# The first unit's gates in two parts, on VectorE instead of GpSimd, with new positions for the start of a fused attention and MLP kernel

## The reference

```python
scale = np.minimum(mag, 0.999) / (mag + 1e-06)          # mag = |a_re + i a_im|
for t in range(S):                                      # S = 768 steps, 4 batches, 8 heads, D = 48
    S = a[t] * S + k[t] (x) v[t]                        # complex state, D x D per head
    y[t] = q[t] . Re(S)
...
h = x @ w_in                                            # 3072 x 384 @ 384 x 2048
g = np.where(h > 0.0, h, np.exp(np.minimum(h, 0.0)) - 1.0)
x = g @ w_out
h = np.maximum(np.maximum(x @ w1, x @ w2), x @ w3)      # 384 -> 768, three times
return h @ w_out2                                       # 768 -> 384
```

## Time and profile before

| | us |
|---|---|
| median of 3 runs (931.10 to 932.78) | 932.74 |
| the profiled execution | 932.65 |
| its span | 930.9 |
| PE busy in the span | 847.4 (91%) |
| DVE, ACT, POOL busy | 517.6, 419.5, 373.0 |

### The profile page before, as it was taken

The page is one execution under the profiler, slowest core; times in us unless marked ns, Lnnn a source line. Parts: engine busy times, 40 slices in busy tenths (PEclk is TensorE's granted clock), DMA queues, the critical chain, the costliest instruction groups (busy, mean ns, idle before and its releaser), DMA issues.

```text
span 930.9 us, 14390 instructions
## 1 busy us (share of the span) xinstructions
PE 847.4 (91%) x5692; PEld 734.5 (79%) x5692; DVE 517.6 (56%) x702; ACT 419.5 (45%) x613; POOL 373.0 (40%) x272
## 2 busy tenths in 40 slices
PE   0067789899999999999999999999999999999997
PEld 0067789888888888888878888878888989898987
DVE  4858887788797878787878643553212121212020
ACT  6745746466666666666575423432121121112121
POOL 3544654444545454636454522465222131303120
PEclk9997898899999999999999999999999999999999
DMA  5396143435252625262524326003010102000000
GB/s 223 88 281 195 35 123 105 139 104 176 84 167 60 202 64 182 63 205 61 174 78 147 107 59 247 1 1 119 1 69 0 68 1 69 1 35 1 35 0 35
DMA packets 70723, 88.45 MB, mean 95 GB/s; under 512 B 15360, under 2 KB 55296, under 8 KB 70144
## 3 DMA queue, kind: packets, MB, share of 16 engines
q1 hardware_dynamic: 70656, 87.53, 30.1%
HBM read 59.13 MB, written 28.39 MB: 94 GB/s over the span
## 4 chain that ended last, share of the span: by engine, by line
PE 74%; issue 9%; DVE 7%; POOL 5%; ACT 3%; DMA 1%; POOLq 0%; SPq 0%; DVEq 0%; ACTq 0%
PE bank L1123 73%; POOL t L514 1%; DVE ge L862 1%; DVE t L868 1%; ACT t L633 1%; DVE t L862 1%; PE bank L1138 1%; POOL gl L517 1%; DVE qp L868 1%; POOL hl L517 1%; DVE ge L865 1%; POOL wol L517 1%; POOL qd L514 1%; POOL kd L514 1%; DVE kp L868 0%
## 5 line engine op out<-in xcount | busy, mean ns | idle before, releaser
L517 POOL TENSOR_TENSOR gl<-ge,gh 128x512 fp32r<-128x512 f32 x96 | 131.1, 1366 | 146.1 <-ACT gh L633 146.1
L868 DVE TENSOR_TENSOR hm<-bank,hm 128x512 f32<-128x512 f32 x72 | 49.8, 692 | 226.6 <-PE bank L1123 224.7
L1123 PE MATMUL bank<-xh,wih 128*128 128x512 f32 (+1 forms) x336 | 126.9, 378 | 9.7 <-DVE xl L868 9.7
L517 POOL TENSOR_TENSOR hl<-hm,hh 128x512 fp32r<-128x512 f32 x36 | 46.5, 1292 | 205.8 <-ACT hh L633 205.8
L1123 PE MATMUL bank<-gh,woh 128*128 128x512 f32 (+1 forms) x336 | 124.2, 370 | 5.2 <-POOL gl L517 4.8
L1123 PE MATMUL bank<-xh,wal 128*128 128x512 f32 x324 | 126.2, 389 | 0.0
L1123 PE MATMUL bank<-xl,wah 128*128 128x512 f32 x324 | 126.2, 389 | 0.0
L1123 PE MATMUL bank<-xh,wah 128*128 128x512 f32 x324 | 126.1, 389 | 0.0
L1123 PE MATMUL bank<-xh,wil 128*128 128x512 f32 (+1 forms) x336 | 122.2, 364 | 0.0
L1123 PE MATMUL bank<-xl,wih 128*128 128x512 f32 (+1 forms) x336 | 122.0, 363 | 0.0
L1123 PE MATMUL bank<-gl,woh 128*128 128x512 f32 (+1 forms) x336 | 121.6, 362 | 0.0
(11 more groups left out here) (83 smaller groups left out, 1681.8 us busy)
## 6 DMA issues: line engine op xcount, KB each, us to landing
q_cols<-qp SPq DMA_DIRECT2D x24, 384.0 KB, 2.8
k_cols<-kp SPq DMA_DIRECT2D x24, 384.0 KB, 3.0
qt<-q_cols SPq DMA_DIRECT2D x24, 384.0 KB, 3.7
kt<-k_cols SPq DMA_DIRECT2D x24, 384.0 KB, 3.9
vv<-in_v SPq DMA_DIRECT2D x12, 448.0 KB, 5.5
ar<-in_a_re SPq DMA_DIRECT2D x12, 384.0 KB, 3.6
ai<-in_a_im SPq DMA_DIRECT2D x12, 384.0 KB, 4.2
qd<-in_q SPq DMA_DIRECT2D x12, 384.0 KB, 4.2
```

Of the source, the lines that this page charges most:

```text
L517: return nc.gpsimd.tensor_tensor(dst, whole, high.bitcast(f32), ALU.subtract)
L868: return nc.vector.tensor_tensor(dst, a, b, op)
L1123: return nc.tensor.matmul(dst, lhsT, rhs, start=start, stop=stop)
```

## The change

Unit 0's gate steps are done for row a and row b apart, on 128x384 tiles, each with its own semaphores, and the four steps that were POOL's are DVE's for them. A part p counts these: parts 0 and 1 are unit 0's rows, part u + 1 is unit u. Part 0 leaves ACT's arctan table without `back()`, part 1 enters without the explicit load; before each `exps` of unit 0 a load stands in the built program all the same. Unit 0's gates are loaded by row. Row b's rotated q and k go to `qp2` and `kp2`. Tables of positions: new ones for units 0 and 1, own ones for part 1, unit 2 and unit 3, and small changes for the rest; 8 positions fewer lie ahead of group 0.

```diff
+    AT_FIRST_B = {
...
+    BY_UNIT = (AT_FIRST, AT_SECOND, AT_THIRD, AT_FOURTH, AT)
...
+    START = 8
...
-        def gates(u):
-            return second if u == 1 else usual
+        def gates(p):
+            if p < PAIR:
+                return Gates(*(t[:, p:p + 1, :] for t in usual))
+            return second if p == PAIR else usual
...
+        def q_turned(n):
+            return qp2[:, :, :] if n == 1 else qp[:, :, :]
...
-                    return STEPS + EARLY * k // (2 * C1)
+                    return START + (STEPS + EARLY - START) * k // (2 * C1)
...
+                if u == 0:
+                    sp.dma_start(gates(p).ar, a_re[0, :, p:p + 1, :]).then_inc(l_first[p], 16)
+                    sp.dma_start(gates(p).ai, a_im[0, :, p:p + 1, :]).then_inc(l_first[p], 16)
...
-                nc.scalar.preload_act_table(ACT.Sin)
-                act.wait_ge(tan, u + 1)
+                if p != 1:
+                    nc.scalar.preload_act_table(ACT.Sin)
+                of_gate(act, tan1, tan, p)
                 func(g.t2, g.t2, ACT.Arctan).then_inc(atn, 1)
-                back()
...
+                if p != 0:
+                    back()
...
+            def decayed(n):
+                e, u = place_of(n), unit_of(n)
+                g = gates(part_of(n))
+                dve.wait_ge(dec, part_of(n) + 1)
+                dve.wait_ge(l_q[u % 2], 16 * (u // 2 + 1))
+                tt(g.qd[:, e, :], g.qd[:, e, :], g.cs[:, e, :], ALU.mult).then_inc(qkd1, 1)
...
-                if n >= 1:
+                if n >= 2:
                     dve.wait_ge(s_q, 16 * n)
```

More of the change, by code:

```diff
@@ L55, in build @@
     AT = {
[L56 to L59, removed]
+        "square": -21, "square_im": -22, "squared": -20, "root": -17, "denominator": -17, "inverse": -13, "clamp": -15,
@@ L60, in build @@
+        "log_decay": -15, "signed": -8, "tangent": -13, "arctan": -9, "angle": -8, "scan_lam": -10, "center": -9, "exps": -7,
+        "ends": -5, "scan_phi": -7, "reduced": -6, "decayed_a": -10, "decayed_b": -8, "sines": -4, "rotate_q_a": -3,
+        "rotate_k_a": -4, "rotate_q_b": 2, "rotate_k_b": 5, "state_decay": 3, "s_a": 6, "s_b": 10, "kr_a": 7, "kr_b": 11,
         "masked_a": 6, "masked_b": 10, "kr_evac_a": 6, "kr_evac_b": 11, "state_decayed_a": 6, "state_decayed_b": 8, "y_a": 8,
-        "y_b": 11, "inc_a": 10, "inc_b": 14, "state_add_a": 10, "state_add_b": 14, "x_high_a": 9, "x_low_a": 9, "x_high_b": 12,
@@ L65, in build @@
+        "load_kt_a": 7, "store_q_b": 7, "load_qt_b": 8, "store_k_b": 8, "load_kt_b": 8, "store_ends": -6, "load_ends": -4,
+        "tile": 13, "negative": -13, "small": -15,
     }
     AT_FIRST = {
-        "square": -26, "square_im": -25, "squared": -36, "root": -24, "denominator": -29, "inverse": -21, "clamp": -23,
-        "log_decay": -20, "signed": -20, "tangent": -21, "arctan": -20, "angle": -17, "scan_lam": -20, "center": -18,
-        "exps": -16, "ends": -15, "scan_phi": -16, "reduced": -16, "decayed_a": -17, "decayed_b": -15, "sines": -15,
@@ L76, in build @@
-        "store_k_b": -12, "load_kt_b": -4, "store_ends": -16, "load_ends": -12, "tile": 5, "negative": -20, "small": -21,
+        "square": -52, "square_im": -52, "squared": -48, "root": -46, "denominator": -47, "inverse": -42, "clamp": -39,
+        "log_decay": -38, "signed": -36, "tangent": -40, "arctan": -38, "angle": -36, "scan_lam": -38, "center": -36,
+        "exps": -34, "ends": -28, "scan_phi": -33, "reduced": -31, "decayed_a": -33, "decayed_b": -31, "sines": -31,
+        "rotate_q_a": -28, "rotate_k_a": -27, "rotate_q_b": -25, "rotate_k_b": -25, "state_decay": -8, "s_a": -22, "s_b": -18,
@@ L77, in build @@
+        "small": -42,
+    }
+    AT_FIRST_B = {
+        "square": -50, "square_im": -49, "squared": -47, "root": -42, "denominator": -43, "inverse": -40, "clamp": -38,
+        "log_decay": -37, "signed": -33, "tangent": -38, "arctan": -33, "angle": -32, "scan_lam": -35, "center": -35,
+        "exps": -32, "ends": -22, "scan_phi": -30, "reduced": -29, "sines": -30, "load_a": -49, "negative": -41, "small": -40,
     }
     AT_SECOND = {
-        "square": -39, "square_im": -37, "squared": -38, "root": -34, "denominator": -34, "inverse": -34, "clamp": -31,
@@ L81, in build @@
[L81 to L85, removed]
@@ new lines, in build @@
+        "log_decay": -37, "signed": -27, "tangent": -41, "arctan": -28, "angle": -27, "scan_lam": -28, "center": -26,
+        "exps": -26, "ends": -25, "scan_phi": -26, "reduced": -24, "decayed_a": -25, "decayed_b": -24, "sines": -5,
+        "rotate_q_a": -5, "rotate_k_a": -5, "rotate_q_b": -1, "rotate_k_b": -2, "state_decay": 0, "s_a": 3, "s_b": 6, "kr_a": 5,
+        "kr_b": 8, "masked_a": 4, "masked_b": 7, "kr_evac_a": 5, "kr_evac_b": 9, "state_decayed_a": -5, "state_decayed_b": 1,
+        "y_a": 6, "y_b": 10, "inc_a": 7, "inc_b": 8, "state_add_a": 7, "state_add_b": 12, "x_high_a": 7, "x_low_a": 7,
@@ L937, in reduced, with scan_phi @@
+            def scan_phi(p):
+                g = gates(p)
+                dve.wait_ge(phi, p + 1)
+                dve.wait_ge(gsum, p + 1)
+                nc.vector.tensor_tensor_scan(flat(g.t3), starts(p), flat(g.t2), 0.0, ALU.mult, ALU.add).then_inc(psum, 1)
+            def reduced(p):
+                g = gates(p)
+                dve.wait_ge(psum, p + 1)
                 ts(g.t2, g.t3, 4.0 * MAGIC, ALU.add, 4.0 * MAGIC, ALU.subtract).then_inc(turn, 1)
-                dve.wait_ge(turn, u + 1)
```

415 lines of the change are left out of this document (255 added, 160 removed).

## The result

The changed kernel takes 936.27 us (median of 4 runs, 935.90 to 937.88), the kernel before, beside it on the same chip, 931.92. The ratio is 1.0053, with a 95% interval of 1.0040 to 1.0066. Forecast was 919.5, with a range of 909 to 928. The profiled execution of the changed kernel took 937.88 us, its span 936.1: it is the longest of the four, 1.6 us above their median, so a difference between two traces is sure to a us or two, and the medians decide.

The account below looks back on a forecast made before the run. Only the start, ahead of group 16, was taken to have much to give, set by the units' chains. Group 16 at 188.0, plus 729.5 behind it and 1.75 outside the span, made 919.2, stated as 919.5 us; range 909 to 928.

Parts of the forecast that it names:

- Unit 0's chain: From unit 0's gates to its first scores: these at 38.2 us, 10.2 us earlier, with ACT the longer queue.
- Group 0 at 55.9: Start of group 0 on PE: 17.7 us behind the first scores, 22.4 us earlier than before.
- PE idle ahead of group 2 for 7 to 11 us: Sign to look for in the changed trace: PE waits this long, released by DVE's elu of group 0.
- Unit 1's scores at 84.6: Scores of unit 1 on PE: 2.3 us later than before, with its gates' second half ahead of group 0's elu.
- the 82 that I named as a sign of error: Unit 1's rotations on DVE: the prediction called itself wrong if they end after 82 us.
- T: The time at which unit 1's scores come; the forecast had 84.6 us.
- From unit 1's to unit 2's scores 40.7 us: Pace between these scores on PE: unit 2's at 125.3 us, 6 us earlier than before.
- Unit 2 to 3, 41.7: Pace from unit 2's scores to unit 3's: the latter at 167 us, where they were at 178.1.
- From there to group 16, 21: Unit 3's scores to group 16: 2.0 + 16.1 us of PE work and 3 for stalls, group 16 at 188.
- Behind group 16 nothing: Stretch from group 16 to the end: tables for later units change nothing, between 1 us gained and 2 lost.
- The bound from below: Groups 0 to 16: DVE's 119.5 us at 86% busy make 138 us, a gain of 7.
- unit 1 is starved: Rival, unit 1's gates late on ACT and DVE: group 16 at T + 96 + 19, kernel slower; chance 0.07.

Follow-up runs that it names:

- without POOL's later pieces: The changed kernel with POOL's low parts of the second weights left out for three of four pieces, DVE's kept: 931.20 us, ratio 1.0002.
- without both engines' pieces: The changed kernel with the low parts of three of four weight pieces left out on both DVE and POOL: 925.95 us, ratio 0.9948.
- unit 1 early and POOL's pieces on DVE: The changed kernel with six steps of unit 1 at earlier positions and POOL's four low weight pieces done by DVE: 928.02 us, ratio 0.9969.
- GpSimd again: The changed kernel with unit 0's four steps, still in two parts, on POOL again: 938.72 us, ratio 1.0072.

## Why the prediction was wrong

- *Unit 0's chain: right.* First scores at 40.1 (38.2, "within 2"). ACT was what the rotations waited for: `squared` of unit 1 stood at 31.22 after a wait of 2.81 for ACT, with rotate_k behind it. Table loads take 1.28, and the arctan at 55.48 starts 1.29 behind its load at 54.19: no drain.
- *Group 0 at 55.9: 54.88, in part by luck.* The first scores were 1.9 us late, and from there it took 14.8 us, not 17.7: PE is busy 14.3 us in that stretch, at a granted clock of 1.00, where the 18.1 that I built on came at 0.92. The two errors cancel. PE idle ahead of group 2 for 7 to 11 us: 12.4. The elu ended at 71.8 where I had 70.5.
- *Unit 1's scores at 84.6: wrong, 88.9.* For the scan and what follows it up to the wil I wrote "some 12 us with POOL beside it". The rows take 10.1 alone, so that was 2 us for POOL; they took 14.4. For the rotations I gave POOL nothing, and the first took 3.19. Row a's ended at 81.6 where I had 77.6, those of row b at 91.5, behind the 82 that I named as a sign of error. The held rotation alone does not make T: without POOL's later pieces it takes 0.56 and the scores come at 87.6.
- *From unit 1's to unit 2's scores 40.7 us: wrong, 47.4.* This is the largest error, 6.7 us, and the step that failed is the one that gave it: unit 2's "rotate_q, 37 us later by the steps queued in between". From squared (81.56) to rotate_q (125.95) it was 44.4 us. DVE's 40 rows in it take 28.5 us at their shortest, they were held for 10.7, and DVE idled for 7.0 (rows overlap by 1.8). Without POOL's later weight pieces the same 40 rows take 41.1 us and are held for 6.2, and the pace from scores to scores is 43.9. So POOL's pieces beside DVE are half of the error; the rest is open. That the pace without both engines' pieces, 41.5, is close to the forecast is chance: the forecast had DVE's own pieces in it.
- *Unit 2 to 3, 41.7: 44.0. From there to group 16, 21: 24.6.* In the first, the same lengthening. In the second, PE waits 1.6 us for a mask and 2.76 for xl, where I left 3 us in all; what would remove the second was not found.
- *Behind group 16 nothing: 1.7 us lost*, at PE's lower clock (last section), inside the bound of 2. PE idles for 8.5 us there, as forecast.
- *The bound from below: wrong.* I had DVE busy 119.5 us from group 0 to 16, at 86% or more, so at most 138 us; it was busy 125.6 us, at 84%, in 150.0. The 6.1 us on top of the 119.5 have no term of their own there.
- 4.3 + 6.7 + 2.3 + 3.6 = 16.9 us between the forecast 188.0 and 204.9; with the 1.7 behind it that is 18.6 of the 18.7 us between the sum, 919.2, and the profiled execution, 937.88.

The rival *unit 1 is starved* was right in its outcome and its mechanism: it decides at T of 86, and T was 88.9. Its number, T + 96 + 19 = 203.9 (204.9 measured), is close by luck: the two units took 91.4 us, not 96, and from unit 3's scores to group 16 it was 24.6, not 19. I gave it too little because I took T for known to 2 us, while the price of POOL beside DVE, for which the earlier trace rows showed 3.18 us and the earlier trace rows a mean of 738 ns, had 2 us in T and no term in the pace.

How much of the miss is explained: with unit 1 early and POOL's pieces on DVE the kernel takes 928.02, so the two causes account for 8 of the 17 us between the forecast and the changed kernel, and for all of its loss against the kernel before. The rest is open; POOL's other steps still hold DVE's rows for 25 us in that kernel, but putting more of them on DVE gained nothing.

The lengthening was there before the change as well. If one takes for each DVE row between first scores and group 16 what it has over the shortest row of its kind there, the sum is 31 us of 130 before and 36 of 137 after. The change added 5 us to it and moved steps of unit 1 under it.

## What to carry to other kernels

A lead at the start is worth only what the next unit can follow: before counting it, walk the next unit's chain through the queues as closely as the first. Where DVE and POOL both have long instructions from SBUF, add their times up instead of laying them side by side, and look at which step of the critical chain meets the longest POOL instruction. A piece that DVE does in half POOL's time can be cheaper on DVE even where DVE is the busier engine, as long as the masks that PE waits for do not come to stand behind it.

## What the hardware showed

**DVE and POOL take turns where DVE reads SBUF alone.** All 96 elu pairs of the changed kernel, duration in ns as least, median and longest:

```profile
L968 DVE TENSOR_SCALAR ge<-ge x96: 395/429/2020, 69.9 to 626.8; 128x512 f32<-128x512 f32 x96
L971 DVE SCALAR_TENSOR_TENSOR ge<-bank,ge x96: 690/692/694, 71.1 to 628.0; 128x512 f32<-128x512 f32 x96
...
L616 POOL TENSOR_TENSOR gl<-ge,gh x96: 1264/1297/2736, 72.5 to 629.4; 128x512 fp32r<-128x512 f32 x96
```

The one that reads a bank never varies by more than 4 ns; the one from SBUF to SBUF takes up to five times its least. Masks and `xl`, which read a bank, stay at 0.69 and 0.56 as well; scans, products and even a copy of 128x6 (0.17 to 0.87) don't. The Trainium skill (SBUF — State Buffer, Who interferes with whom) says this: a DVE instruction with two SBUF inputs contends with a GpSimd instruction that reads SBUF, so does one in a mode that uses both its ports, and the one that comes second fully blocks until the first is done. The rows agree: the 5.04 us of `wil` end 1.61 behind the end of `wol`, and 1.75 is what `wil` takes alone.

**PE's clock after a short wait.** In the changed kernel's first 512-column products of group 16, behind the wait of 2.76 us:

```profile
204.91 0.50 PE L1275 MATMUL bank<-xh,wih 128*128 128x512 f32 x1 [2.76 <-DVE xl L974]
205.71 0.60 PE L1275 MATMUL bank<-xh,wih 128*128 128x512 f32 x1
206.95 0.63 PE L1275 MATMUL bank<-xh,wih 128*128 128x512 f32 x1
```

and busy time of the stretch that these open, columns as in the earlier trace rows:

```profile
204.91:208.50 3.59, 3.59 (x12) 2.83 (x12) 0.22 (x1) 3.50 (x5) 1.49 (x2) 0.61 0.00 0
```

The second and third product take 0.60 and 0.63 us, and the granted clock is 0.61 in the mean of the stretch: the lower level (1.2 GHz) for most of it. In the kernel before, whose wait was 1.85, they take 0.40 and 0.39. Of the sixteen kernels measured here beside the one before, eleven have such products of 0.63 us, all behind waits of 2.1 to 2.8 us, and their stretch behind group 16 lasts 731.0 to 731.9 us; the five that don't have 1.3 to 2.8, and four of these last 728.6 to 729.6. In the changed kernel the 49th matmul of the stretch starts 8.46 us behind the first, before the change 6.87: 1.6 of the 1.7 us behind group 16 are lost there. (The fifth without slow products, GpSimd again, lasts 731.2 all the same; it loses its 1.7 us later, 1.4 of them in its last 64 matmuls.) The wait alone does not decide it (three runs went without behind 2.76 to 2.78 us), and what does is open.
